# Quarter-array score products, POOL pooling in half pieces and another load order in a fused attention and mixture kernel

## The chip, the cores and the metric

The kernel runs on one core of one Trainium2 chip. The metric is the device time of one execution in microseconds; lower is better. TensorE is called PE here, VectorE DVE, ScalarE ACT, GpSimd POOL; SP is the engine that only issues DMAs.

## What is computed

Three stages follow one another. The sizes are B = 8, H = 8, S = 576 queries and keys, head size 64, keys and values averaged over groups of 8 (72 pooled keys), N = B*S = 4608 tokens of width 512.

```python
k_p, v_p = k.reshape(B,H,72,8,64).mean(3), v.reshape(B,H,72,8,64).mean(3)
attn = softmax((q @ k_p.T) / 8)                      # 1e-9 added to each sum
x = (attn @ v_p)                                     # tokens x 512
logits = x @ phi                                     # 32 slots
d, c = softmax(logits, 0), softmax(logits, 1)        # 1e-9 added to each sum
slot_out = per expert: relu((d.T @ x) @ w1) @ w2     # 8 experts, 4 slots each
x = c @ slot_out
out = (s * relu(x @ w_in)**2 + b) @ w_out            # width 512 -> 2048 -> 512
```

## The kernel before, in words

The program is written by hand, one instruction stream per engine, with semaphores between them. The first part (attention, logits, and the sums over tokens that softmax over tokens needs) runs over 36 **units** of 128 queries by 4 heads (every ninth step holds a **mixed** unit, 64 queries of each of two batches by 8 heads), nine units for each of four **pairs** of batches. It is a pipeline in numbered **steps** `n`; each engine walks the same steps in its own program order. In step n PE does, in this order: the fold of the logits of unit n-5 (L1209), the scores of unit n-1 (L1231, or L1225 if the unit is mixed), the transposes of the queries of unit n (L1264), the logits of unit n-4 (L1292, L1287), the transposes of the weights of unit n-3 (L1305), then what belongs to a pair: turns of pooled keys and values (L1147), the product of the values with phi (L1170, `values_phi`), values back to natural order (L1179), and the sums over tokens (L1334 to L1342, L1352, L1361, L1366), once in two halves for each of 8 batches. L1193 are products whose results nobody reads; they stand only in the last steps.

DVE takes the row maximum of the scores in PSUM (L944, `mx`), sums the exponentials of the unit before (L980, `den`), subtracts the maximum into SBUF (L987, `ex`), takes reciprocals (L991), and pools keys (L897, with a second copy of the result by L901). The scores of the next unit wait for that subtraction (`sx_ready`), as they use the same two PSUM banks. ACT exponentiates and copies PSUM to SBUF: queries (L702), keys (L709), values (L718), weights (L725), transposed attention weights (L799). All turns and the queries share PSUM bank 0, so the queries of a step wait until ACT has kept what was turned in the step before.

POOL normalises a unit (L678, `normalise`; step n takes unit n-2, PE transposes that unit in step n+1) and pools key and value pieces: a first addition halves a piece of 8 rows to 4 (L664, 128x768), a second to 2 (L664, 128x384), and two more write the result twice (L671). `pool_pieces(n)` says which whole pieces POOL takes behind the normalisation of step n; `dve_keys(n)` says which thirds of a key piece DVE takes. A pair has three key and three value pieces of 768 KB; the buffer `kvbuf` holds three of the pieces at a time (RING), in the order of `KV_ORDER`. Per later pair DVE pools two key pieces and POOL one key and three value pieces.

SP issues every DMA in program order (L559 to L600), and a wait before one holds all that follow: a `kvbuf` load waits until the piece three places earlier in `KV_ORDER` is pooled, a load of queries until the transposes have read the buffer. The 2 MB expert matrices stand between them.

Behind the 36 units come the expert products (L1389, L1410), and from about 260 us to the end the last two products (L1439, L1455 to L1457), which the change doesn't touch.

The arrays are named in the order of the streams below. A score product of an ordinary unit and one of the mixed unit read in the code:

```python
last = pe.matmul(bank[S_B[j]][:, KEYS * a:KEYS * (a + 1)], qT[rows, a, :], k_sb[...], ...)        # L1231, rows = 64 of 128
last = pe.matmul(bank[S_B[h % 2]][toks, KEYS * (h // 2):...], qT[rows, h // 2, toks], k_sb[...], ...)  # L1225, toks = 64 of 128
```

## Time and profile before

| | us |
|---|---|
| median of 3 runs (lowest, highest) | 707.23 (701.81, 719.14) |
| the profiled execution | 703.28 |
| its span | 701.4 |
| busy: PE, its weight loads, DVE, ACT, POOL | 667.3, 526.2, 384.2, 326.7, 103.4 |
| mean granted clock of PE, of full speed | 0.976 |

A row of a timeline or of a chain of waits begins with its start and its length in us; then come engine, line, operation, what is written and read (partitions x elements), and how many instructions it merges; in brackets the idle time before it and what ended it. PE shows two records for most products in fp32 and one for a transpose, and the records overlap: the length of a row runs on past the start of the next, so a PE piece is taken from start to start. A table of stretches has the stretch, its length, the busy time of PE, weight loads, DVE, ACT and POOL with their instructions, the granted PE clock (1.00 is 2.4 GHz, 0.50 is 1.2 GHz), the DMA share and GB/s. In the page's slices a digit is tenths busy of one fortieth of the span, 17.5 us.

### The profile page before, as it was taken

What the parts mean: (1) busy time and instruction counts of PE and PEld (TensorE: products, weight loads), DVE (VectorE), ACT (ScalarE), POOL (GpSimd) and SP (SyncE); (2) the same over time, 40 slices, a digit from 0 to 9 for tenths busy, and PEclk for the clock granted to TensorE, in tenths of its full rate; (3) what the DMA queues carried; (4) which work ended last, traced back from release to release, by engine and by line L of the source; (5) the groups of instructions that cost most, each with busy time, mean ns of one, the idle gap of its engine ahead of it and who ended that gap; (6) DMA issues with size and microseconds to landing.
All of it is one profiled execution on the core that took longest, in us unless ns stands there. A gap on an engine that the chain in (4) does not pass through costs nothing.

```text
span 701.4 us, 12092 instructions
## 1 busy us (share of the span) xinstructions
PE 667.3 (95%) x4618; PEld 526.2 (75%) x4618; DVE 384.2 (55%) x631; ACT 326.7 (47%) x607; POOL 103.4 (15%) x106
## 2 busy tenths in 40 slices
PE   6759999999998889999999999999999999999996
PEld 6647788787774335888888888888888888888885
DVE  6437777756534566665445454454554544544542
ACT  1436767776631226554444444444444444444442
POOL 2556565662211000000000000000000000000000
PEclk9778999999999999999999999999999999999999
DMA  9948878555257991001001010010010000100101
GB/s 334 325 124 302 315 268 300 183 158 209 90 215 279 427 428 78 0 1 60 1 10 52 1 40 20 0 60 0 0 60 0 30 30 0 61 0 1 61 0 60
DMA packets 25228, 80.37 MB, mean 115 GB/s; under 512 B 6496, under 2 KB 14688, under 8 KB 22368
## 3 DMA queue, kind: packets, MB, share of 16 engines
q1 hardware_dynamic: 25184, 79.76, 30.8%
q8 instruction: 30, 0.49, 0.3%
q14 instruction: 14, 0.11, 0.0%
HBM read 70.32 MB, written 9.44 MB: 114 GB/s over the span
## 4 chain that ended last, share of the span: by engine, by line
PE 88%; POOL 3%; DVE 3%; DMA 2%; ACT 1%; issue 1%; ACTq 0%; SPq 0%; DVEq 0%; POOLq 0%
PE bank L1455 19%; PE bank L1457 19%; PE bank L1456 19%; PE bank L1305 5%; PE bank L1439 5%; PE bank L1231 4%; PE bank L1264 2%; PE bank L1292 2%; POOL kvbuf L664 2%; PE bank L1389 2%; DMA kvbuf<-in_v_dram 2%; PE bank L1410 2%; PE bank L1334 1%; PE bank L1209 1%; PE bank L1352 1%
## 5 line engine op out<-in xcount | busy, mean ns | idle before, releaser
L1455 PE MATMUL bank<-w_hi,r_hi 128*128 128x512 f32 x576 | 224.2, 389 | 1.4 <-DVE r_lo L1093 1.4
L1457 PE MATMUL bank<-w_hi,r_lo 128*128 128x512 f32 x576 | 224.1, 389 | 0.0
L1456 PE MATMUL bank<-w_lo,r_hi 128*128 128x512 f32 x576 | 224.1, 389 | 0.0
L1087 DVE SCALAR_TENSOR_TENSOR win_sb<-win_sb,sb_col 128x512 f32<-128x512 f32 x144 | 108.5, 753 | 196.8 <-ACT win_sb L840 196.8
L840 ACT ACTIVATE win_sb<-bank 128x512 f32<-128x512 f32 x144 | 86.1, 598 | 217.8 <-PE bank L1439 217.8
L1455 PEld LDWEIGHTS bank<-w_hi,r_hi 128*128 128x128 f32 x576 | 108.1, 188 | 24.4 <-DVE r_lo L1093 2.0
L1457 PEld LDWEIGHTS bank<-w_hi,r_lo 128*128 128x128 f32 x576 | 108.1, 188 | 22.5
L1456 PEld LDWEIGHTS bank<-w_lo,r_hi 128*128 128x128 f32 x576 | 108.1, 188 | 22.4
L1093 DVE SCALAR_TENSOR_TENSOR r_lo<-win_sb,sb_col,r_hi 128x512 fp32r<-128x512 f32 x144 | 107.7, 748 | 1.5 <-ACT r_hi L849 1.5
L849 ACT ACTIVATE r_hi<-win_sb,sb_col 128x512 fp32r<-128x512 f32 x144 | 103.2, 717 | 1.6 <-PE bank L1457 1.6
L1439 PE MATMUL bank<-cT,g_st 128*128 (+1 forms) x144 | 56.4, 393 | 0.0
L799 ACT ACTIVATE aT<-bank 72x512 f32<-72x512 f32 x72 | 39.1, 588 | 29.5 <-PE bank L1305 29.4
L678 POOL TENSOR_TENSOR ex<-ex,den 128x576 f32<-128x576 f32 x36 | 41.3, 1149 | 70.8 <-DVE den L991 70.8
L1305 PE MATMUL bank<-ident,ex 128*72 128x128 f32 x288 | 40.8, 287 | 8.9 <-POOL ex L678 8.9
L1305 PEld LDWEIGHTS bank<-ident,ex 128*72 128x72 f32 x288 | 30.7, 120 | 22.3 <-issue 11.5
L664 POOL TENSOR_TENSOR kvbuf<-kvbuf 128x768 f32<-128x768 f32 (+1 forms) x30 | 42.2, 1406 | 24.2 <-DMA kvbuf<-in_v_dram 17.6
L944 DVE TENSOR_REDUCE mx<-bank 128x8 f32<-128x576 f32 x36 | 27.2, 757 | 30.5 <-PE bank L1231 29.5
L1231 PE MATMUL bank<-k_sb,qT 64*128 64x72 f32 x512 | 37.4, 288 | 0.1
L702 ACT ACTIVATE qT<-bank 128x512 f32<-128x512 f32 x36 | 21.5, 597 | 34.2 <-PE bank L1264 34.0
L1231 PEld LDWEIGHTS bank<-k_sb,qT 64*128 64x128 f32 x512 | 32.7, 196 | 2.4 <-issue 1.0
L1439 PEld LDWEIGHTS bank<-cT,g_st 128*128 128x128 f32 x144 | 26.9, 188 | 6.6 <-DVE g_st L1073 0.8
L897 DVE TENSOR_REDUCE kp<-kvbuf 128x64 f32<-128x512 f32 x24 | 24.2, 1024 | 7.9 <-DMA kvbuf<-in_k_dram 7.9
(137 smaller groups left out, 577.4 us busy)
## 6 DMA issues: line engine op xcount, KB each, us to landing
early_third<-in_moe_w_dram SPq DMA_DIRECT2D x6, 2048.0 KB, 13.4
kvbuf<-in_k_dram SPq DMA_DIRECT2D x12, 768.0 KB, 6.0
kvbuf<-in_v_dram SPq DMA_DIRECT2D x12, 768.0 KB, 5.2
out_dram<-win_sb SPq DMA_DIRECT2D x36, 256.0 KB, 2.3
qbuf<-in_q_dram SPq DMA_DIRECT2D x8, 1024.0 KB, 8.6
early<-in_moe_w_dram SPq DMA_DIRECT2D x4, 2048.0 KB, 10.2
late<-in_moe_w_dram SPq DMA_DIRECT2D x4, 2048.0 KB, 17.4
win_sb<-in_moe_w_in_dram SPq DMA_DIRECT2D x4, 1024.0 KB, 4.8
```

The source lines that it names most:

```text
L664: pool.tensor_tensor(buf[:, :, 0:width], buf[:, :, 0:width], buf[:, :, width:2 * width], ALU.add).then_inc(pool_step, 1)
L678: pool.tensor_tensor(e, e, r, ALU.mult).then_inc(a_ready, 1)
L840: act.activation(r_sb[:, n % 2, :], bank[4 + n % 2][:, :], ACT.Relu).then_inc(r_ready, 1)
L849: act.activation(r2_hi[:, n % 2, :], g_sb[:, n % 2, :], ACT.Identity, bias=sb_col[:, 1:2]).then_inc(hi_ready, 1)
L1087: dve.scalar_tensor_tensor(out=g_sb[:, n % 2, :], in0=r_sb[:, n % 2, :], scalar=sb_col[:, 0:1], in1=r_sb[:, n % 2, :], op0=ALU.mult, op1=A ...
L1093: dve.scalar_tensor_tensor(out=r2_lo[:, n % 2, :], in0=g_sb[:, n % 2, :], scalar=sb_col[:, 1:2], in1=r2_hi[:, n % 2, :].bitcast(F32), op0= ...
L1231: last = pe.matmul(bank[S_B[j]][:, KEYS * a:KEYS * (a + 1)], qT[rows, a, :], k_sb[i % 2][rows, H * bb + HB * unit_half(U) + a, :], start=T ...
L1305: last = pe.transpose(bank[A_B[g]][0:KEYS, P * a:P * (a + 1)], ex[:, U % EXR, HB * g + a, 0:KEYS], ident[:, :])
L1439: pe.matmul(bank[4 + f % 2][:, :], g_st[:, P * f:P * (f + 1)], cT[:, bass.ds(c * CH, CH)], start=True, stop=True).then_inc(h_ready, 1)
L1455: pe.matmul(acc, r2_hi[:, f % 2, toks], w_hi[:, f, :], start=(f == 0), stop=False)
L1456: pe.matmul(acc, r2_hi[:, f % 2, toks], w_lo[:, f, :], start=False, stop=False)
L1457: last = pe.matmul(acc, r2_lo[:, f % 2, toks], w_hi[:, f, :], start=False, stop=(f == F2C - 1))
```

## The change

- **Scores**: each score product of an ordinary unit is split into two with 64 query columns each, so that four products at 64 rows by 64 columns stand in a row, as in the mixed unit.
- **Small products**: the fold of the logits (L1209) and the turn of the token sums (L1352) are split by output partitions too (64 and 64; 64 and 8). The broadcast of the running maximum (L1246) takes all 128 rows instead of 32.
- **Denominator**: the two products with a column of ones (L1340, L1342) go. The matrix of token sums takes the 73rd column of `ex`, which holds 1e-9, with it, and the later step divides by 1e-9.
- **POOL**: a piece is pooled in two parts (`halve`, and `pool_rest` with the other three additions), which stand in different steps, and POOL takes two of the three key pieces of a later pair; DVE pools one.
- **Loads**: `KV_ORDER` is keys then values for every pair; the value pieces of pair 1 are issued ahead of the first matrix.
- **Start**: the last value piece of pair 0 is turned one step later, and its product with phi too, through another PSUM bank.
- **DVE**: two copies from SBUF to SBUF (L901, L1010) are written as reductions over one element.

```diff
         def weights_step(i):
-            return TPP * i + 2 if i else 3
+            return TPP * i + 2 if i else 4
...
-                steps = (2, 3, 4, 5, 6, 6) if i == 1 else tuple(TPP * i - 9 + x for x in (0, 1, 2, 4, 5, 6))
-                at += [(i, 2 * (x // GP), x % GP) for x in range(2 * GP) if steps[x] == n]
+                steps = (3, 4, 4) if i == 1 else tuple(TPP * i - 10 + g for g in range(GP))
+                at += [(i, 0, g) for g in range(GP) if steps[g] == n]
...
-                steps = (3, 5, 6, 8) if i == 1 else tuple(TPP * i - 7 + 2 * x for x in range(4))
-                at += [(i, *((1, 0), (0, 1), (1, 1), (1, 2))[x]) for x in range(4) if steps[x] == n]
+                steps = (3, 4, 4, 5, 5, 6, 6, 7, 7, 8) if i == 1 else tuple(TPP * i - 10 + x for x in range(10))
+                pieces = ((0, 1), (0, 2), (1, 0), (1, 1), (1, 2))
+                at += [(pieces[x // 2][0], i, pieces[x // 2][1], x % 2) for x in range(10) if steps[x] == n]
...
+            for u in range(PIECES):
+                load_kv(1, 1, u)
             load_matrix(0)
-            load_kv(1, 1, 0)
             load_q(1, 0)
             load_q(1, 2)
...
-                dve.tensor_copy(pm[:, 1:, :], pm[:, 0:1, :].to_broadcast([P, QUADS, SLOTS])).then_inc(pm_ready, 1)
+                dve.reduce_max(pm[:, 1:, :], pm[:, 0:1, :].to_broadcast([P, QUADS, SLOTS]).unsqueeze(3), AX.X).then_inc(pm_ready, 1)
...
-                        last = pe.matmul(bank[MISC][:, SLOTS * j:SLOTS * (j + 1)], l4[:, l4_cols(U)][:, P * j:P * (j + 1)], fold[:, 0, :],
-                                         start=True, stop=True)
+                        for half, toks in parts():
+                            first = P * j + HALF * half
+                            last = pe.matmul(bank[MISC][toks, SLOTS * j:SLOTS * (j + 1)], l4[:, l4_cols(U)][:, first:first + HALF],
+                                             fold[:, 0, :], start=True, stop=True)
...
-                                last = pe.matmul(bank[S_B[j]][:, KEYS * a:KEYS * (a + 1)], qT[rows, a, :],
-                                                 k_sb[i % 2][rows, H * bb + HB * unit_half(U) + a, :], start=True, stop=True)
+                                for _, toks in parts():
+                                    last = pe.matmul(bank[S_B[j]][toks, KEYS * a:KEYS * (a + 1)], qT[rows, a, toks],
+                                                     k_sb[i % 2][rows, H * bb + HB * unit_half(U) + a, :], start=True, stop=True)
...
-                    if half == 0:
-                        pe.matmul(found[:, DEN:DEN + 1], dl[:, g % 2, 0:QT, :].rearrange("p j s -> p (j s)"), ones[:, :],
-                                  start=False, stop=True, skip_group_check=True)
-                        last = pe.matmul(found[0:QUAD, DEN:DEN + 1], dl[:, g % 2, QT, :], ones[:, :],
...
-                        last = pe.matmul(bank[B_B][0:KEYS, SLOTS * h:SLOTS * (h + 1)], b_sb[:, h // HB, KEYS * x:KEYS * (x + 1)], fold[:, 0, :],
-                                         start=True, stop=True)
+                        for keys in (slice(0, HALF), slice(HALF, KEYS)):
+                            last = pe.matmul(bank[B_B][keys, SLOTS * h:SLOTS * (h + 1)],
+                                             b_sb[:, h // HB, LANES * x + keys.start:LANES * x + keys.stop], fold[:, 0, :],
```

**POOL, its first normalisations.** In the rows below `ex<-ex,den` is the normalisation of a unit and the others are additions of one piece (`kp` a key piece, `vp` a value piece). Before, a whole value piece stands behind the second normalisation:

```order
L678 TENSOR_TENSOR ex<-ex,den 128x8x72 x2
L664 TENSOR_TENSOR kvbuf<-kvbuf 128x3x256
L664 TENSOR_TENSOR kvbuf<-kvbuf 128x3x128
L671 TENSOR_TENSOR vp<-kvbuf 128x3x64 x2
L678 TENSOR_TENSOR ex<-ex,den 128x8x72 x2
```

Now the first addition of a key piece stands there, and from then on two parts of different pieces between two normalisations:

```order
L677 TENSOR_TENSOR ex<-ex,den 128x8x72 x2
L657 TENSOR_TENSOR kvbuf<-kvbuf 128x3x256
L677 TENSOR_TENSOR ex<-ex,den 128x8x72
L664 TENSOR_TENSOR kvbuf<-kvbuf 128x3x128
L670 TENSOR_TENSOR kp<-kvbuf 128x3x64 x2
L657 TENSOR_TENSOR kvbuf<-kvbuf 128x3x256
L677 TENSOR_TENSOR ex<-ex,den 128x8x72
```

The value piece of pair 1 moved behind both key pieces and two more normalisations.

**PE, steps 3 and 4.** `kp` and `vp` are turned pieces, `k_sb,qT` scores, `qbuf` queries, `ident,ex` transposed weights, `phi_bd,vT` the product with phi, `aT,vphi` logits. Before:

```order
L1147 MATMUL bank<-ident,vp 128x128 x6
L1231 MATMUL bank_2<-k_sb,qT 128x72 x8
L1264 MATMUL bank<-ident,qbuf 128x128 x4
L1305 MATMUL bank<-ident,ex 72x128 x8
L1170 MATMUL bank<-phi_bd,vT 72x64 x8
L1231 MATMUL bank_2<-k_sb,qT 128x72 x8
```

Now:

```order
L1146 MATMUL bank<-ident,vp 128x128 x3
L1235 MATMUL bank_2<-k_sb,qT 64x72 x16
L1268 MATMUL bank<-ident,qbuf 128x128 x4
L1311 MATMUL bank<-ident,ex 72x128 x8
L1146 MATMUL bank<-ident,vp 128x128 x3
L1235 MATMUL bank_2<-k_sb,qT 64x72 x16
L1268 MATMUL bank<-ident,qbuf 128x128 x4
L1169 MATMUL bank<-phi_bd,vT 72x64 x8
L1298 MATMUL bank<-aT,vphi 32x256 x4
```

A score group is 16 products instead of 8; one turn of values and the product with phi moved down, the latter to just ahead of the first logits.

**SP, behind the key pieces of pair 1.** `early` is an expert matrix. Before:

```order
L537 DMA kvbuf<-in_k_dram 128x1536 x3
L557 DMA early<-in_moe_w_dram 128x4096
L537 DMA kvbuf<-in_v_dram 128x1536
L546 DMA qbuf<-in_q_dram 128x8x256
```

Now:

```order
L540 DMA kvbuf<-in_k_dram 128x1536 x3
L540 DMA kvbuf<-in_v_dram 128x1536 x3
L560 DMA early<-in_moe_w_dram 128x4096
L549 DMA qbuf<-in_q_dram 128x8x256
```

The matrix and the next queries moved behind all three value pieces.

## Rows read from the trace of the kernel before

**Rows 1.** The page: span, and the granted clock in 40 slices.

```profile
span 701.4 us, 12092 instructions
...
PEclk9778999999999999999999999999999999999999
```

**Rows 2.** Busy time by stretch: steps 11 to 36, and one pair of batches.

```profile
72.41:190.04 117.63, 117.22 (x1582) 93.69 (x1581) 79.77 (x166) 82.18 (x178) 59.97 (x58) 1.00 0.61 217
82.38:125.13 42.75, 42.58 (x571) 34.25 (x571) 31.23 (x63) 29.94 (x66) 25.58 (x26) 1.00 0.76 267
```

**Rows 3.** The chain of waits, 36 to 49 us.

```profile
36.67 0.93 DVE kp L897
...
37.94 4.49 DMA kvbuf<-in_v_dram
...
42.51 1.80 POOL kvbuf L664
...
44.38 1.00 POOL kvbuf L664
...
45.45 1.13 POOL vp L671 x2
46.59 1.11 POOL ex L678
```

**Rows 4.** Timeline of POOL, 42 us.

```profile
42.51 2.87 POOL L664 TENSOR_TENSOR kvbuf<-kvbuf 128x768 f32<-128x768 f32 x2 [9.73 <-DMA kvbuf<-in_v_dram]
```

**Rows 5.** Timeline of PE: steps 2, 5 and 11.

```profile
26.42 0.90 PE L1147 MATMUL bank<-ident,vp 128*128 128x128 f32 x3 [3.03 <-POOL vp L671]
...
47.75 1.92 PE L1305 MATMUL bank<-ident,ex 128*72 128x128 f32 x8 [8.55 <-POOL ex L678]
...
74.94 1.07 PE L1305 MATMUL bank<-ident,ex 128*72 128x128 f32 x8
```

**Rows 6.** Busy time and clock by stretch, 28 to 60 us.

```profile
28.00:30.00 2.00, 2.00 (x16) 1.87 (x15) 0.65 (x1) 0.71 (x2) 0.00 (x0) 0.50 0.98 313
...
44.00:48.00 4.00, 0.25 (x2) 0.23 (x3) 0.00 (x0) 0.00 (x0) 3.84 (x6) 0.50 0.57 117
...
58.00:60.00 2.00, 2.00 (x22) 1.42 (x21) 1.84 (x3) 1.37 (x4) 1.92 (x2) 1.00 0.74 187
```

**Rows 7.** Timeline of DVE, step 5.

```profile
38.18 0.76 DVE L944 TENSOR_REDUCE mx<-bank 128x8 f32<-128x576 f32 x1 [0.26 <-PE bank L1225]
...
40.18 0.19 DVE L991 RECIPROCAL den<-den 128x8 f32<-128x8 f32 x1
```

**Rows 8.** The page, DMA issues: queries; KB each, us to landing.

```profile
qbuf<-in_q_dram SPq DMA_DIRECT2D x8, 1024.0 KB, 8.6
```

**Rows 9.** Timeline of PE, steps 12 to 16.

```profile
81.12 0.31 PE L1337 MATMUL bank<-ex,dl 128*32 128x72 f32 x8
81.36 0.38 PE L1340 MATMUL bank<-ones,dl 128*128 128x1 f32 x2
...
81.82 0.63 PE L1209 MATMUL bank<-fold,l 128*128 128x32 f32 x4
82.38 1.11 PE L1231 MATMUL bank<-k_sb,qT 64*128 64x72 f32 x16
83.43 0.66 PE L1264 MATMUL bank<-ident,qbuf 128*128 128x128 f32 x4
...
86.77 0.73 PE L1225 MATMUL bank<-k_sb,qT 64*64 64x72 f32 x32
87.43 0.33 PE L1240 MATMUL bank<-ident,pm 128*128 128x128 f32 x1
...
89.92 1.17 PE L1352 MATMUL bank<-fold,b_sb 128*72 128x32 f32 x16
...
97.09 0.63 PE L1264 MATMUL bank<-ident,qbuf 128*128 128x128 f32 x4 [0.17 <-ACT k_sb L709]
```

**Rows 10.** One line of DVE: the copy of the maxima.

```profile
L1010 DVE COPY pm<-pm x8: 226/700/990, 68.3 to 206.9; 128x128 f32<-128x128 f32 x8
```

More of the change, by code:

```diff
@@ L398, in value_bank @@
         def value_bank(i, u):
-            return bank[Q_B if i or u < 2 else B_B]
+            return bank[Q_B]
         def natural_bank(i, half):
@@ L406, in first_query_bank @@
             keys = [(i, u) for i in range(1, PAIRS) for u in range(PIECES) if key_step(i, u) == n]
-            values = [(i, u) for i in range(PAIRS) for u in range(PIECES) if value_step(i, u) == n and (i or u < 2)]
-            weights = [i for i in range(PAIRS) if weights_step(i) == n]
+            values = [(i, u) for i in range(PAIRS) for u in range(PIECES) if value_step(i, u) == n]
+            weights = [i for i in range(1, PAIRS) if weights_step(i) == n]
             naturals = [(i, h) for i in range(PAIRS) for h in range(2) if natural_step(i, h) == n and (i or h == 0)]
@@ L654, in _, with halve, pool_rest @@
                                pattern=[[-1, P]], channel_multiplier=1).then_inc(consts, 1)
-            pool.memset(ones[:, :], 1.0).then_inc(consts, 1)
             pool.memset(phi_bd[:, :, :], 0.0).then_inc(phi_zero, 1)
-            def pool_piece(which, i, u, piece):
+            PARTS = [(which, 0, u, part) for which, u in ((0, 1), (1, 1), (1, 2)) for part in range(2)]
+            PARTS += [part for n in range(STEPS) for part in pool_parts(n)]
+            def halve(which, i, u):
                 slot, loads = kv_piece(which, i, u)
+                buf = kvbuf[:, slot]
                 pool.wait_ge(kv_in[slot], 16 * loads)
+                pool.tensor_tensor(buf[:, :, 0:ROW // 2], buf[:, :, 0:ROW // 2], buf[:, :, ROW // 2:ROW], ALU.add).then_inc(pool_step, 1)
+            def pool_rest(which, i, u):
+                slot, loads = kv_piece(which, i, u)
                 buf = kvbuf[:, slot]
-                for n, width in enumerate((ROW // 2, ROW // 4)):
-                    pool.tensor_tensor(buf[:, :, 0:width], buf[:, :, 0:width], buf[:, :, width:2 * width],
-                                       ALU.add).then_inc(pool_step, 1)
-                    pool.wait_ge(pool_step, 2 * piece + n + 1)
+                pool.wait_ge(pool_step, PARTS.index((which, i, u, 0)) + 1)
+                pool.tensor_tensor(buf[:, :, 0:ROW // 4], buf[:, :, 0:ROW // 4], buf[:, :, ROW // 4:ROW // 2], ALU.add).then_inc(pool_step, 1)
+                pool.wait_ge(pool_step, PARTS.index((which, i, u, 1)) + 1)
                 if i:
@@ L678, in normalise @@
                 pool.tensor_tensor(e, e, r, ALU.mult).then_inc(a_ready, 1)
-            POOLED = [piece for n in range(STEPS) for piece in pool_pieces(n)]
-            pool_piece(0, 0, 1, 0)
-            pool_piece(1, 0, 1, 1)
-            pool_piece(1, 0, 2, 2)
+            for which, u in ((0, 1), (1, 1), (1, 2)):
+                halve(which, 0, u)
+                pool_rest(which, 0, u)
             for n in range(STEPS):
@@ L686, in _ @@
                     normalise(n - 2)
-                for i, which, u in pool_pieces(n):
-                    pool_piece(which, i, u, 3 + POOLED.index((i, which, u)))
+                for which, i, u, part in pool_parts(n):
+                    (halve, pool_rest)[part](which, i, u)
             pool.wait_ge(b_ready, 2 * B)
@@ L1314, in _ @@
                 for i in range(PAIRS):
-                    if n == weights_step(i):
+                    if i and n == weights_step(i):
                         values_phi(i, n)
```

104 lines of the change are left out of this document (50 added, 54 removed).

## The prediction

> **What bounds the kernel now.** I read the page first: a span of 701.4 us, with PE at its full clock except near the start, where the digits fall to 7 and 8 [rows 1]. The part from about 260 us on is not touched. So the question is the first 218 us, and I cut them by stretches. From 72.41 to 190.04 us (steps 11 to 36) PE is busy for 117.22 of 117.63 us at clock 1.00, and in one pair of batches, nine steps, for 42.58 of 42.75 us; DVE has 31.23 us there, ACT 29.94, POOL 25.58 [rows 2]. That stretch is bound by PE: what PE no longer does there is gained, until another engine's round trip takes over.
>
> The beginning is different. The chain of waits shows a DVE reduction of keys at 36.67 us, then a value piece's DMA of 4.49 us, three kinds of POOL additions, and only then, at 46.59, the normalisation that PE needs [rows 3]. POOL had stood idle for 9.73 us for that value piece [rows 4], with the normalisation queued behind it, and PE lost 8.55 us to it [rows 5]. PE also pays afterwards: the clock is 0.50 at 44 to 48 us and 1.00 again at 58 to 60 [rows 6]. A wait of 3.03 us at step 2 [rows 5] is followed in the same way by 0.50 at 28 to 30 us [rows 6].
>
> **Part A, the start (to the transposes of unit 8 in step 11).** The profile of a changed start must be worked out anew along its slowest engine, which I take to be POOL. Up to the scores of unit 4 I give nothing: turning the last value piece one step later takes the wait of 3.03 us out of step 2, but the normalisation of unit 0 still stands behind all three first pieces on POOL, so about 3 us of PE idle and the half clock come back in step 3; and the phi product, now just ahead of the logits that need it, adds one round trip over ACT. So DVE's maximum for unit 4 stays at 38.18 us and its reciprocal ends at 40.18 + 0.19 = 40.4 [rows 7]. From there POOL has no reason to pause: keys 1 and 2 of the pair are loaded by then, and the first value piece, issued when DVE has pooled its keys at about 38, needs 4.49 us to land [rows 3], while POOL reaches it only at 43.7. From the chain a first halving takes 44.38 - 42.51 = 1.87 us, the rest of a piece 46.59 - 44.38 = 2.21, a normalisation 1.11 [rows 3]. Between 40.4 and the release of unit 8 stand six normalisations (3 to 8), the rests of five pieces and the halvings of four: 6 x 1.11 + 5 x 2.21 + 4 x 1.87 = 25.2 us, so unit 8 is released at 65.6 and its transposes start at about 65.7, against 74.94 [rows 5]. Part A gives **9.2 us**. POOL's own work grew here (a key piece of 1.87 + 2.21 = 4.1 us more); the gain is that the DMA wait is gone. Late next is POOL itself.
>
> Bounds of part A. Above: the whole PE wait, 8.55 us, and half of the roughly 10 us at half clock (44 to 56 us), 5 us, and five score groups of 0.39, as derived below: 15.5. Below: the queries of pair 1 are now behind the first matrix and all three value pieces. Value piece 3 waits for key piece 3 to be pooled (40.4 + 1.11 + 2.21 = 43.7), then 0.8 + 2.1 + 1.0 MB follow; at the 313 GB/s of one row [rows 6] that is 12.5 us, and 8.6 us is the median for such a load [rows 8], so they land between 52 and 56. PE wants them at about 54: the normalisation of unit 5 ends at 40.4 + 3 x 1.11 + 2 x 2.21 + 2 x 1.87 = 51.9, and its transposes, a turn and the next scores lie between. The key piece behind them holds DVE for some us too, under POOL's chain. If both break through that cover and the clock falls again, some 5 us go: lower bound 4.
>
> **Part B, steps 12 to 36.** A score group of an ordinary unit takes 83.43 - 82.38 = 1.05 us, the mixed unit's, with the same number of output values and four quarter arrays, 87.43 - 86.77 = 0.66 [rows 9]. The new groups have that form, row halves and column halves in the same order. 22 of the 25 groups here are ordinary: 22 x 0.39 = 8.6 us. Against it: where keys were turned a step earlier, the queries already wait 0.17 us for ACT's copy of them [rows 9], so shorter scores only lengthen that wait. I take that once for each of two pairs, 0.8, and as much again for the other copies that ACT makes out of bank 0: 7.0 us remain. DVE is no hindrance: from its maximum to the end of the subtraction 40.18 - 38.18 = 2.0 us pass [rows 7], while PE has over 3 us of other work in a step of 42.75 / 9 = 4.75 us [rows 2]. POOL would have 9 x 1.11 + 5 x 4.08 = 30.4 us per pair where PE keeps over 38; cover enough.
>
> The products with ones go: 81.82 - 81.36 = 0.46 us for each batch [rows 9], six here: 2.8 us. The column that replaces them lies in products that run anyway. The logits' fold takes 82.38 - 81.82 = 0.56 us [rows 9], 11 double and 3 single ones here, 12.5 in all; the turn of the token sums takes 1.17 at most [rows 9] and, without the overlap of its last record, 1.0, six of them. No row shows these two in their new form. At best they shorten like the scores (by 0.37 of their length): 2.6 and 2.2 us. At worst each of the doubled records takes as long as a present one, which doubles both: a loss of 7 and 6. The nearest row is the column-split group of L1337, 8 records of 72 columns in 81.36 - 81.12 = 0.24 us, 30 ns each [rows 9], against 65 ns for each of the 16 records of an ordinary score group with the same 72 columns; so neighbours in other columns do overlap, and I take a third of the best: 0.9 and 0.7. Part B: 7.0 + 2.8 + 0.9 + 0.7 = **11.4 us**, bounds 5 and 16.
>
> The Trainium skill ("TensorE: Matmul & The Clock Gate", Part 3, The mechanism) says that weight loads overlap running matmuls only where their row groups differ. The two small products keep all 128 rows and split columns only; by that rule nothing is gained on them, and by its reading at its harshest the doubled records are paid in full. The 30 ns of the row above speak against the harsh reading.
>
> **Part C, the last steps and the start's small change.** Two more batches without the ones products: 0.9 us. The copy of the maxima takes 226 to 990 ns [rows 10]; its long cases lie beside POOL additions, and in the last steps PE waits for it. As a reduction I take the short value always and 0.5 us off the path. The remaining folds and turns give 0.4. Part C: **1.8 us**, bounds 0.5 and 3.
>
> The Trainium skill ("SBUF — State Buffer", on the port that DVE and GpSimd share) says the same of the copy: a copy can take the shared port pair and block against GpSimd, a reduction on this chip never does. By it the 0.5 us is safe; without it the copy would have stayed between the two values of the row.
>
> Behind the last steps the expert products wait for matrices whose loads are started by PE's own progress, so the gain passes through. Sum: 9.2 + 11.4 + 1.8 = 22.4; the span becomes 679.0. The profiled execution took 703.28, 1.9 more than its span, so 680.9, rounded to **681 us**. That is 3.2% below its own execution and 3.7% below the median of 707.23; the runs shown reach from 701.81 to 719.14.
>
> **Rivals.**
> 1. *The start gives little.* PE waits for POOL in short pieces all the way and runs them at half clock, or queries land late. For it: every PE wait of 3 us so far was followed by 0.50. Against: the new waits are about 1 us each. Part A falls to 4: 686 us.
> 2. *Another round trip takes the steady steps.* ACT's copies out of bank 0, or DVE, hold every step, or the quarter products with the same keys twice are no faster than halves. For it: the 0.17 us. Against: 1.1 us of other PE work stand in most such places. The 7.0 us go: 688 us.
> 3. *The column-split small products are paid by the record.* 7 + 6 lost instead of 1.6 gained in part B, and 3.5 in part C (two folds and two turns doubled, 3.1, instead of the 0.4): 681 + 18 = 699 us, no difference.
> 4. *POOL is starved again, once per pair.* Three places of the piece buffer and one issue queue: if a load lands a step (4.75 us) later than POOL's program wants it, the normalisation behind it is held as at 42.51. A wait like that cost 8.55 us and about 5 of half clock; in each of pairs 1 to 3 that is 3 x 13.5 = 41 us: 681 + 41 = 722 us, slower. It decides where the wait costs over 22.4 / 3 = 7.5 us per pair. For it: the second key piece of pair 2 can be issued only when a value piece is pooled, one step ahead of its own halving. Against: in pairs 2 and 3 almost all other pieces have two steps, 9 us, for a landing of 4.49.
>
> **How the numbers follow.** Chances: forecast 0.62, rival 1 0.14, rival 2 0.14, rival 3 0.06, rival 4 0.04. The measurement can tell about 2% from no change, so the border is 693 us. The forecast and rivals 1 and 2 lie below it, save a small part at their upper ends; faster 0.86, within 2% 0.10, slower 0.04. The range takes in rivals 1 and 2 with some room, and below the better half of the bounds of A and B: 670 to 693.
>
> **What would show it.** POOL: no wait for a value piece's DMA above 1 us before 60 us, and the transposes of unit 8 at 64 to 68 us. Scores: 0.66 us from start to start in every group. One pair of batches: 42.75 - 4 = 38.5 to 39 us, PE still full, with waits of queries for ACT up to 0.6 us once or twice per pair. Folds below 0.56 and turns of token sums below 1.0 us; above those, rival 3. Copies of the maxima as reductions near 0.25 us. I would be wrong in part A if PE's clock stayed at 0.50 past 45 us or a queries' wait of more than 2 us stood at step 9, and in part B if the pair took more than 41 us.

## The result: no faster, and where the 30 us went

The changed kernel takes 710.79 us (median of 14 runs, 706.79 to 715.48); the kernel before took 702.92 on the same chip (14 runs, 699.43 to 719.14). The ratio of the two is 1.012, with a 95% interval of 1.009 to 1.014: slower, by less than the 2% that stood as the border. Three of the 14 executions of the kernel before (714 to 719 us) are slow ones, at a lower clock, such as any kernel shows now and then; the ratios here and below leave them out. The forecast was 681, range 670 to 693. The profiled execution of the changed kernel is its slowest, 715.48 us with a span of 713.7, so the two traces lie 12.3 us apart where the medians lie 7.9 apart; the stretches below carry that excess.

I cut both traces, and the forecast, at the same four places. Starts in us, from the timelines of PE; the third column is the forecast's own arithmetic (74.94 - 9.2, then the stretches of before less 11.4 and 1.8).

| | before | after | forecast |
|---|---|---|---|
| transposes of unit 8 (step 11) | 74.94 | 70.40 | 65.7 |
| scores of step 36 | 190.04 | 193.53 | 169.4 |
| first expert product | 218.26 | 229.72 | 195.8 |
| end of the span | 701.4 | 713.7 | 679.0 |

So the start gained 4.5 us instead of 9.2, the steady steps lost 8.0 instead of gaining 11.4, the last steps lost 8.0 instead of gaining 1.8, and the rest is longer by 0.8 (483.98 us instead of 483.14). The page of the changed kernel shows the new trouble in one line; it answers to [rows 1], and a digit is one fortieth of 713.7 us:

```profile
span 713.7 us, 13446 instructions
...
PEclk9896999999795999999999999999999999999999
```

In the kernel before the clock had been full from the fifth slice on. Now there is a 6 in the fourth, a 7 at 178 to 196 us and a 5 at 214 to 232, and the windows below find more. They answer to [rows 2, 6] and have the same columns (the clock is the third number from the end):

```profile
44.00:48.00 4.00, 2.59 (x80) 1.98 (x78) 2.42 (x5) 2.64 (x6) 4.00 (x5) 1.00 0.99 419
...
60.00:68.00 8.00, 6.14 (x60) 4.35 (x62) 6.99 (x15) 3.51 (x8) 7.21 (x7) 0.50 0.94 360
70.40:193.53 123.13, 119.64 (x1998) 88.93 (x1994) 67.91 (x151) 80.66 (x174) 61.26 (x60) 0.93 0.56 195
95.00:105.00 10.00, 10.00 (x182) 7.17 (x185) 4.03 (x8) 7.11 (x15) 5.03 (x5) 0.83 0.27 82
175.00:185.00 10.00, 10.00 (x134) 7.60 (x137) 3.00 (x7) 3.71 (x10) 2.04 (x2) 0.63 0.25 104
193.53:229.72 36.19, 34.99 (x381) 25.69 (x377) 9.81 (x30) 9.56 (x24) 5.52 (x5) 0.80 0.47 175
```

At 44 to 48 us, where the kernel before waited at clock 0.50, PE now works at 1.00: the wait for the value piece is gone. But 60 to 68 us is at 0.50, and the stretch from step 11 to 36, which had 1.00 throughout, has a mean of 0.93. PE is listed as busy for the whole of 175 to 185 us while it runs at a mean of 0.63. A busy PE is not a quick PE.

The instruction that costs the most is found by walking PE's timeline from start to start, as in [rows 9]:

```profile
103.42 0.31 PE L1212 MATMUL bank<-fold,l 128*64 128x32 f32 x4
103.66 0.73 PE L1235 MATMUL bank<-k_sb,qT 64*64 64x72 f32 x32
104.32 0.66 PE L1268 MATMUL bank<-ident,qbuf 128*128 128x128 f32 x4
...
106.81 3.17 PE L1357 MATMUL bank<-fold,b_sb 128*64 128x32 f32 x32
109.90 0.29 PE L1235 MATMUL bank<-k_sb,qT 64*64 64x72 f32 x4
```

Scores take 104.32 - 103.66 = 0.66 us, as forecast. The turn of the token sums takes 109.90 - 106.81 = **3.09 us** (3.10 in others) where it took 1.0 to 1.1 before; its 32 records come every 97 ns, against 69 ns for each of the 16 before. (Its row names only the first of its two shapes.) There are eight such turns: five in the steady stretch, three in the last steps. The forms of line L1357, and who waits for it:

```profile
L1357 PE MATMUL bank<-fold,b_sb x256: 193/222/317, 84.2 to 225.2; 128*64 128x32 f32 x64, 128*8 128x32 f32 x64
...
  ACT bT L766: 22.2, 8
```

The last of the eight even runs at half clock and takes 225.37 - 220.89 = 4.5 us.

The other small products did well: the fold of the logits takes 0.35 us for a double one (99.51 - 99.16, below) instead of 0.56, and the half-sums that had carried the products with ones take 0.75 instead of 1.21:

```profile
97.81 1.20 PE L1340 MATMUL bank<-ex,dl 128*32 128x292 f32 x8
98.79 0.44 PE L1345 MATMUL bank<-ex,dl 128*32 128x73 f32 x8
99.16 0.42 PE L1212 MATMUL bank<-fold,l 128*64 128x32 f32 x8
99.51 0.73 PE L1235 MATMUL bank<-k_sb,qT 64*64 64x72 f32 x32
...
102.67 0.70 PE L1340 MATMUL bank<-ex,dl 128*32 128x292 f32 x8
103.18 0.31 PE L1345 MATMUL bank<-ex,dl 128*32 128x73 f32 x8
103.42 0.31 PE L1212 MATMUL bank<-fold,l 128*64 128x32 f32 x4
```

(0.75 is 103.42 - 102.67; the group at 97.81 falls partly into a half-clock stretch.)

At the start, POOL's wait of 9.73 us [rows 4] and PE's of 8.55 [rows 5] are gone, and others stand in their place. From the timelines of PE, DVE and POOL, 55 to 62 us:

```profile
55.25 1.11 PE L1268 MATMUL bank<-ident,qbuf 128*128 128x128 f32 x4 [4.89 <-DMA qbuf<-in_q_dram]
...
61.86 1.24 PE L1235 MATMUL bank<-k_sb,qT 64*64 64x72 f32 x32 [1.99 <-DVE ex L986]
```

```profile
58.59 1.03 DVE L896 TENSOR_REDUCE kp<-kvbuf 128x64 f32<-128x512 f32 x1 [10.83 <-DMA kvbuf<-in_k_dram]
```

```profile
60.50 1.81 POOL L657 TENSOR_TENSOR kvbuf<-kvbuf 128x768 f32<-128x768 f32 x1 [5.29 <-DMA kvbuf<-in_k_dram]
```

Three engines wait for a transfer at once: PE for the queries of step 9, DVE and POOL for the first key piece of pair 2. DVE's wait is not idle time that costs nothing: the subtraction of step 9's scores is queued behind that reduction, and the 1.99 us of PE is for it. All three transfers stand behind the first 2 MB matrix on the one issue queue.

### The profile page after: what moved, and what is told of

It is laid out like the page before. It is cut to its first block, busy times and chain, and to the rows that moved or that the text cites. A ratio compares the mean times of both kernels' runs of the same rounds, so it can differ in the third digit from the quotient of the medians.

```text
span 713.7 us, 13446 instructions
## 1 busy us (share of the span) xinstructions
PE 679.6 (95%) x5298; PEld 523.6 (73%) x5298; DVE 372.0 (52%) x619; ACT 326.9 (46%) x607; POOL 114.7 (16%) x117
## 4 chain that ended last, share of the span: by engine, by line
PE 84%; DMA 7%; DVE 3%; POOL 2%; issue 2%; ACT 1%; ACTq 0%; DVEq 0%; POOLq 0%
PE bank L1461 18%; PE bank L1462 18%; PE bank L1463 18%; PE bank L1445 4%; PE bank L1311 4%; DMA late<-in_moe_w_dram 4%; PE bank L1357 4%; PE bank L1298 2%; PE bank L1235 2%; PE bank L1268 2%; DMA kvbuf<-in_k_dram 2%; PE bank L1395 2%; PE bank L1340 2%; PE bank L1194 1%; POOL kvbuf L657 1%
## 5 line engine op out<-in xcount | busy, mean ns | idle before, releaser
L1311 PE MATMUL bank<-ident,ex 128*72 128x128 f32 x288 | 43.1, 299 | 2.2 <-POOL ex L677 2.2
L1268 PE MATMUL bank<-ident,qbuf 128*128 128x128 f32 x144 | 26.1, 310 | 11.8 <-DMA qbuf<-in_q_dram 8.0
L657 POOL TENSOR_TENSOR kvbuf<-kvbuf 128x768 f32<-128x768 f32 x18 | 32.6, 1811 | 15.7 <-DMA kvbuf<-in_k_dram 10.6
L1235 PE MATMUL bank<-k_sb,qT 64*64 64x72 f32 x1024 | 25.8, 242 | 3.2 <-DVE ex L986 3.0
L1268 PEld LDWEIGHTS bank<-ident,qbuf 128*128 128x128 f32 x144 | 18.2, 160 | 14.3 <-DMA qbuf<-in_q_dram 8.4
```

Source lines behind the costliest of these rows:

```text
L1235: last = pe.matmul(bank[S_B[j]][toks, KEYS * a:KEYS * (a + 1)], qT[rows, a, toks], k_sb[i % 2][rows, H * bb + HB * unit_half(U) + a, :], s ...
L1268: last = pe.transpose(bank[Q_B][:, P * a:P * (a + 1)], src, ident[:, :])
L1311: last = pe.transpose(bank[A_B[g]][0:KEYS, P * a:P * (a + 1)], ex[:, U % EXR, HB * g + a, 0:KEYS], ident[:, :])
```

## The experiments

Twelve kernels, in four groups of runs: 1 to 4, 5 to 8, 9 to 11, and 12. Each ratio is to the kernel before in the same group (medians of 701.0, 703.1, 702.5 and 702.9 us). As these medians differ by 2 us, kernels of two groups are compared more safely by their ratios. Two theories stood at first: the split turn costs the time, by itself and by the clock behind it; or the start does, since its waits leave half clock behind them. Behind each stands what was expected of it, as it was written before the run.

**1. a_turn_whole: the turn of the token sums as one product again, all else as changed**

```diff
-                        for keys in (slice(0, HALF), slice(HALF, KEYS)):
+                        for keys in (slice(0, KEYS),):
```

> The changed kernel, but the turn of the token sums is one product of 72 output rows again (with the new column stride). Theory 1, the split turn costs 2.1 us for each of eight batches (3.10 against 1.01 us from start to start), and the low clocks that follow it cost more: the turn takes 1.0 us, eight turns give back 17 us, the stretches at 0.50 behind turns go too, 2 to 6 us; run 688 to 692 us where the changed kernel is at 710.8. Rival, the turn only fills time in which PE would wait for something else (POOL, ACT) anyway: under 8 us come back, run above 703.

684.86 us (683.85 to 686.33), ratio 0.978 (0.974 to 0.982). One line of the code is worth 25.9 us between the medians, 24 by the ratios (1.012 - 0.978 of 702.9). Timeline of PE and windows (steps 11 to 36; the last steps):

```profile
99.82 1.17 PE L1357 MATMUL bank<-fold,b_sb 128*72 128x32 f32 x16
100.92 0.73 PE L1235 MATMUL bank<-k_sb,qT 64*64 64x72 f32 x32
```

```profile
67.55:172.38 104.83, 101.92 (x1918) 78.67 (x1914) 67.95 (x151) 80.37 (x174) 61.44 (x60) 1.00 0.66 234
...
172.38:198.27 25.89, 23.44 (x333) 18.25 (x329) 9.80 (x30) 9.59 (x24) 5.53 (x5) 0.99 0.62 229
```

The steady stretch falls from 123.13 to 104.83 us and its clock rises from 0.93 to 1.00; the last steps fall from 36.19 to 25.89, the clock from 0.80 to 0.99. The five turns of the steady stretch, 2.0 us each, are 10.0 of its 18.3; PE's waits for "issue" (below) fall from 2.3 to 0.9, 1.4 more; the other 7 are left for the stretches at half clock, which are gone with the split turn though no other instruction differs. The clock column allows at most (1 - 0.93) x 123.13 = 8.6 us for them. The low clock went with the turn.

**2 and 3. a_turn_grouped and a_turn_32: the same split in another order, and in pieces of 32, 32 and 8 rows**

```diff
-                    for h in range(H):
-                        x = h % HB
-                        for keys in (slice(0, HALF), slice(HALF, KEYS)):
+                    for keys in (slice(0, HALF), slice(HALF, KEYS)):
+                        for h in range(H):
+                            x = h % HB
```

> The changed kernel, the same 16 split products of the turn, but first all eight with 64 output rows, then all eight with 8. Theory 1a, what costs is the change between a 64-column and an 8-column piece at each product (97 ns per record): with one change left the turn takes 0.5 to 0.9 us and the run is at 687 to 692. Rival 1b, each doubled record that fills all 128 rows costs by itself, because its weight load cannot run under a product in the same rows: the turn stays at 3.1 us, the run at 711. Rival 1c, the 8-column pieces are slow in themselves: about half of the loss stays, turn 1.8 to 2.4 us, run 698 to 704.

688.15 us (687.59 to 689.84), ratio 0.982 (0.979 to 0.985).

```diff
-                        for keys in (slice(0, HALF), slice(HALF, KEYS)):
+                        for keys in (slice(0, QUAD), slice(QUAD, HALF), slice(HALF, KEYS)):
```

> The changed kernel, the turn in three parts of 32, 32 and 8 output rows, alternating as before, 48 records. Theory 1a, the cost lies in the change of piece size between 64-column and 32-column tiles, and 8 columns count as a 32-column tile: no change is left, the turn takes 0.7 to 1.3 us, run 688 to 693. Rival 1b (records cost by themselves, 97 ns): 48 x 97 = 4.7 us, run 724. Rival 1c (8 columns slow in themselves): turn 2 us or more.

685.86 us (684.65 to 686.96), ratio 0.978 (0.975 to 0.982). PE's timelines, of the grouped kernel first:

```profile
102.07 1.68 PE L1357 MATMUL bank<-fold,b_sb 128*64 128x32 f32 x32
103.68 0.73 PE L1235 MATMUL bank<-k_sb,qT 64*64 64x72 f32 x32
```

```profile
100.70 0.70 PE L1357 MATMUL bank<-fold,b_sb 128*32 128x32 f32 x48
101.33 0.73 PE L1235 MATMUL bank<-k_sb,qT 64*64 64x72 f32 x32
```

The same 32 records take 3.10 us when pieces of 64 and 8 columns alternate and 1.61 us when all of one width come first; in 32, 32 and 8, as many as 48 records take 0.63 us, 13 ns each. So neither the number of records nor the split as such is dear: the alternation of 64 with 8 is. The grouped order saves 1.49 us and has one change of width where the other has fifteen, so a change costs about 1.49 / 14 = 0.11 us. That is an estimate, which takes it that the records cost the same otherwise. The grouped turn itself took longer than the 0.5 to 0.9 us expected of it, 50 ns a record, and that no run explains. The pieces of 32, 32 and 8 alternate too and pay nothing of the kind; the reading that fits all three is that 8 and 32 columns use the array in the same division and 64 and 8 do not. It is argued from these three orders; no run tries other pairs of widths.

The Trainium skill ("TensorEngine Tiling (Array Packing)", Tiling Modes, Key Properties) says that a change of tiling mode, not of the tile within one, drains the engine; the three orders agree with it, and add the price. Another sentence of it ("TensorE: Matmul & The Clock Gate", Part 3, The mechanism), that a weight load overlaps running products only where its row groups differ, does not agree: 13 ns per record was measured among products that all use the same 128 rows, and the weight loads of kernel 3's turns are 85 to 113 ns long each, so in a turn of 0.63 us they must overlap.

**4. a_queries_first: the queries of pair 1 ahead of the first matrix, the split turn kept**

```diff
-            load_matrix(0)
             load_q(1, 0)
             load_q(1, 2)
+            load_matrix(0)
```

> The changed kernel with the queries of pair 1 issued ahead of the first expert matrix instead of behind it; the split turn stays. Theory 2, the matrix of 2 MB held up the queries (PE idle 4.89 us at 50 us) and, less, the first key piece of pair 2 (DVE idle 10.83 us): the wait for queries goes, that for the key piece stays in part since the matrix is still ahead of it; 2 to 5 us come back, run 706 to 709. Rival, DMA bandwidth is the limit whatever the order: queries wait less, the key piece waits as long or longer, under 1 us comes back.

708.77 us (702.53 to 711.18), ratio 1.010 (1.004 to 1.017): within the 706 to 709 expected, but it can't be told from 710.79. PE's wait for the queries of step 9 is gone, and its wait for DVE grew to take its place:

```profile
61.80 1.24 PE L1235 MATMUL bank<-k_sb,qT 64*64 64x72 f32 x32 [6.04 <-DVE ex L986]
```

DVE still waits 9.5 us for its key piece of pair 2. Unit 8's transposes start at 70.03, against 70.40. Of two transfers that are late together, moving one gives nothing that these runs can measure.

**5. b_turn_split: the kernel before, with only the turn of the token sums split**

```diff
-                        last = pe.matmul(bank[B_B][0:KEYS, ...], b_sb[:, h // HB, KEYS * x:KEYS * (x + 1)], fold[:, 0, :],
-                                         start=True, stop=True)
+                        for keys in (slice(0, HALF), slice(HALF, KEYS)):
+                            last = pe.matmul(bank[B_B][keys, ...], b_sb[:, h // HB, KEYS * x + keys.start:KEYS * x + keys.stop], fold[:, 0, :],
+                                             start=True, stop=True)
```

> The kernel before with one thing of the change: the turn of the token sums split into 64 and 8 output rows, alternating. Theory 1, the alternation costs by itself, whatever else is changed: the turn goes from 1.0 to 3.1 us, eight of them are 17 us, and low clocks behind it add 2 to 8: 720 to 726 us where the kernel before is at 701 to 703. Rival, it costs only beside the new scores (whose pieces are 64 by 64): turn 1.0 to 1.5 us, under 705.

735.31 us (731.46 to 742.43), ratio 1.048 (1.039 to 1.058): some 30 us (28.3 between the two profiled spans), more than the 19 to 25 expected. The turn is the same as in the changed kernel, and so is what follows:

```profile
109.43 3.17 PE L1353 MATMUL bank<-fold,b_sb 128*64 128x32 f32 x32
112.53 1.12 PE L1231 MATMUL bank<-k_sb,qT 64*128 64x72 f32 x16
```

```profile
60.00:190.00 130.00, 129.61 (x1520) 100.29 (x1519) 78.38 (x163) 79.88 (x170) 62.63 (x60) 0.91 0.60 207
```

Eight turns at 2.0 us are 16; a clock of 0.91 where it was 1.00 carries the rest, (1 - 0.91) x 130 = 11.7 us. PE has hardly a wait there that could be blamed: 0.9 us in all between 60 and 225 us. The clock is 0.74 at 89.4 to 96 us, 0.58 at 138 to 146, 0.54 at 162 to 176 and 0.69 at 190 to 201, each directly behind a split turn; behind the turn that ends at 112.53 it is 1.00. Taken from the changed kernel the split gives about 25 back, added to the one before it costs about 30: one cause, seen from both sides.

**6. b_scores: the kernel before, with only the quarter scores**

```diff
-                                last = pe.matmul(bank[S_B[j]][:, KEYS * a:KEYS * (a + 1)], qT[rows, a, :],
-                                                 k_sb[i % 2][rows, H * bb + HB * unit_half(U) + a, :], start=True, stop=True)
+                                for _, toks in parts():
+                                    last = pe.matmul(bank[S_B[j]][toks, KEYS * a:KEYS * (a + 1)], qT[rows, a, toks],
+                                                     k_sb[i % 2][rows, H * bb + HB * unit_half(U) + a, :], start=True, stop=True)
```

> The kernel before with the quarter-array scores alone. Theory, the scores are worth 0.39 us in each of 32 ordinary groups, less where ACT or POOL ends the step: 7.0 of 8.6 us in steps 12 to 36 and up to 1.5 at the start: 692 to 695 us. Rival, another engine's round trip takes the place of the shorter scores: above 698.

694.74 us (694.52 to 696.08), ratio 0.988 (0.983 to 0.993): 8.4 us from the scores alone. In the steady stretch, 71.47 to 182.46 us, it is 115.1 - 111.0 = 4.1; PE's own busy time there fell by 7.3, and its waits grew from 0.4 us to 3.6; the longest:

```profile
PE bank L1265 <- DMA qbuf<-in_q_dram: 1.8, 1, 1.8
PE bank L1265 <- ACT k_sb L709: 1.1, 2, 0.6
```

The other half of the gain lies in the start, 3.5 us, and the last steps.

**7. c_matrix_later: turn in 32s, queries first, and the first matrix behind the key pieces of pair 2**

```diff
-            load_matrix(0)
             load_q(1, 0)
             load_q(1, 2)
             for i in range(2, PAIRS):
                 for u in range(PIECES):
                     load_kv(0, i, u)
+                if i == 2:
+                    load_matrix(0)
                 load_matrix(2 * i - 3)
```

> The changed kernel with the turn in parts of 32, 32 and 8, and the first expert matrix issued behind the key pieces of pair 2, so behind the queries of pair 1 too. Theory 2, the 2 MB of the matrix make both waits at step 8 and 9 (queries 2.8 to 6.6 us, key piece 10 us, which in its turn holds DVE and so the scores): with the matrix away the piece has only the queries before it, DVE's wait falls below 4 us, PE's below 1.5, and the half clock that follows goes: 5 to 9 us below the 685.9 of the turn in 32s, 677 to 681. Rival, the piece is late because its place in the buffer comes free late (issued at 48 us, wanted at 48): DVE still waits 5 us or more and under 3 us come back.

684.78 us (684.19 to 687.58), ratio 0.974 (0.969 to 0.980). Unit 8's transposes start at 62.45 instead of 68.81 in kernel 3, and yet, where 5 to 9 us were expected, the time differs by only 1.1 us between the medians and 2.7 by the ratios: of the 6.4 us, 3.5 are left at step 36 (173.15 against 176.64) and 2.8 in the span (682.4 against 685.2). DVE's wait for the key piece fell from 10.31 to 4.32 us, short of the theory's 4; and PE now waits 3.65 us for POOL ahead of the transposes at 78.81.

**8. c_whole_pieces: the same, with POOL pooling whole pieces**

```diff
-                steps = (3, 4, 4, 5, 5, 6, 6, 7, 7, 8) if i == 1 else tuple(TPP * i - 10 + x for x in range(10))
+                steps = (3, 3, 4, 4, 5, 5, 6, 6, 7, 7) if i == 1 else tuple(TPP * i - 10 + x // 2 * 2 for x in range(10))
```

> As the run before, but POOL pools each piece whole behind one normalisation (4.1 us in one go, every second step) instead of in two parts. Theory, halves only keep a normalisation from waiting 2 us in places where PE has less than that in hand: in steps of about 4 us one unit in two is late by up to 1 us for 27 steps, 2 to 8 us slower than with the halves. Rival, the order of the loads did all the work and halves are worth nothing: same within 1.5 us.

685.85 us (684.13 to 692.33), ratio 0.978 (0.970 to 0.985): not to be told from kernel 7, where 2 to 8 us more were expected. PE waits 6.0 us for POOL between 40 and 75 us instead of 2.9, and unit 8 is later by 0.9. The two parts of a piece give nothing that can be measured.

**9. d_whole_later: kernel 7 with the turn whole**

> The changed kernel with the turn of the token sums whole and the first expert matrix behind the key pieces of pair 2. In the changed kernel with the whole turn the transposes of unit 8 start at 67.6 us, with the matrix moved at 62.5. Theory, PE's program has become long enough for its time that it now and then waits for its own instructions (gaps ended by nothing but issue, six in the run with 48 records per turn, one with 16, none before), and these gaps ate the 5 us in the run with the matrix moved: with 16 records per turn there are at most two such gaps and the 5 us stay: 679 to 682 us. Rival, gaps come with the faster start whatever the number of records: four gaps or more, 683 to 686.

683.76 us (681.41 to 686.28), ratio 0.974 (0.968 to 0.980). The edits are that of kernel 1 and the move of the matrix in kernel 7. Unit 8 starts at 61.88, and the scores of step 36 at 174.24: later than in kernel 1, which had started 5.7 us after it. PE waits 3.65 us for POOL at 78.08, with half clock behind it, and has only 0.35 us of "issue". So it is not that the gaps of kernel 7 ate the start's gain; the stall had moved, and kernel 7 has the same one. The 679 to 682 expected did not come, nor did the rival's four gaps.

**10. d_keys_step9: the same, DVE takes its first third of the keys of pair 2 a step later**

```diff
-                steps = (3, 4, 4) if i == 1 else tuple(TPP * i - 10 + g for g in range(GP))
+                steps = (3, 4, 4) if i == 1 else (9, 9, 10) if i == 2 else tuple(TPP * i - 10 + g for g in range(GP))
```

> As the run before, and DVE pools the first third of the first key piece of pair 2 in step 9 instead of step 8. Theory, DVE's wait of 4.3 us for that piece (landing at 52.3 us) is a wait of a program that asks too early; one step later it has landed: DVE's wait under 0.5 us, PE's wait of 0.86 for the scores goes, 0.5 to 2 us faster than the run before. Rival, DVE then has two thirds in step 9 beside the maxima and holds the next scores instead: same or slower.

684.08 us (683.13 to 686.25), ratio 0.976 (0.971 to 0.980). DVE's wait is gone and the time is the same. POOL and PE show why:

```profile
74.70 1.80 POOL L658 TENSOR_TENSOR kvbuf<-kvbuf 128x768 f32<-128x768 f32 x1 [7.34 <-DMA kvbuf<-in_v_dram]
```

```profile
77.66 1.92 PE L1312 MATMUL bank<-ident,ex 128*72 128x128 f32 x8 [3.77 <-POOL ex L678]
```

The piece that POOL waits for is a value piece of pair 2, and it now stands behind two matrices, 4 MB.

**11. d_fold_whole: kernel 9 with the fold of the logits whole again**

```diff
-                        for half, toks in parts():
-                            first = P * j + HALF * half
-                            last = pe.matmul(bank[MISC][toks, SLOTS * j:SLOTS * (j + 1)], l4[:, l4_cols(U)][:, first:first + HALF],
-                                             fold[:, 0, :], start=True, stop=True)
+                        last = pe.matmul(bank[MISC][:, SLOTS * j:SLOTS * (j + 1)], l4[:, l4_cols(U)][:, P * j:P * (j + 1)], fold[:, 0, :],
+                                         start=True, stop=True)
```

> As the first run of this call, with the logits' fold as one product of 128 output rows again instead of 64 and 64. By the traces the split fold takes 0.36 us where the whole one took 0.56 (double ones) and 0.24 against 0.34 (single ones), 16 and 4 of them: 16 x 0.20 + 4 x 0.10 = 3.6 us, less where a step's end is set by ACT: 2 to 3.6 us slower than the first run of this call. Rival, only its records shrink and the steps are set elsewhere: same within 1 us.

683.85 us (682.68 to 689.14), ratio 0.976 (0.969 to 0.983), against 683.76. The split fold is 0.2 us shorter in each step, and the 2 to 3.6 us that this should give are not seen; runs that spread over 6 us would not show one or two.

**12. e_one_matrix: kernel 10 with the matrices issued one at a time**

```diff
-                if i == 2:
-                    load_matrix(0)
-                load_matrix(2 * i - 3)
+                if i > 2:
+                    load_matrix(i - 2)
                 load_q(i - 1, 1)
                 for u in range(PIECES):
                     load_kv(1, i, u)
-                load_matrix(2 * i - 2)
                 load_q(i, 0)
                 load_q(i, 2)
+                load_matrix(0 if i == 2 else 2)
             load_q(PAIRS - 1, 1)
+            load_matrix(3)
+            load_matrix(4)
```

> d_keys_step9 with the expert matrices issued one at a time between the pieces of keys, values and queries of pairs 2 and 3, so that the value piece of pair 2 no longer lies behind two matrices (4 MB). Theory (a matrix ahead of a piece is what the engines wait for at the start): POOL's wait of 7.3 us for the value piece of pair 2 near 75 and TensorE's 3.8 us behind it fall under 2 us, the stretch of half clock behind them goes, and the time is 3 to 6 us below the 684.1 of d_keys_step9: 678 to 681. Rival (the start's transfers only choose which piece is late; the data wanted by then is the same): the wait comes back at a later pair or at the expert products' matrices, and the time is within 2 us of d_keys_step9, 682 to 686.

**679.98 us** (677.53 to 680.83), ratio 0.966 (0.964 to 0.969): the fastest of all, 22.9 us below the kernel before and 30.8 below the changed one. No engine waits for a piece of pair 2 any more; POOL's waits from 60 to 90 us are for DVE's reciprocals, 2.15 us at most. Page and windows (the steady stretch, the last steps):

```profile
span 679.0 us, 13190 instructions
...
PEclk9699999999988999999999999999999999999999
```

```profile
64.25:169.28 105.03, 101.83 (x1918) 78.60 (x1914) 67.96 (x151) 80.29 (x174) 62.71 (x61) 1.00 0.75 274
169.28:195.16 25.88, 23.43 (x332) 18.24 (x328) 9.79 (x30) 9.56 (x24) 5.52 (x5) 0.99 0.63 230
```

Unit 8 starts here at 64.25, later than in kernels 9 and 10 (61.88, 61.03); what counts is that nothing stalls behind it. The matrices were not late at the expert products: PE waits 1.55 us for DVE ahead of the first, as in the kernel before.

## Why the prediction was wrong, step by step

**Part B, the turn of the token sums: the step that failed.** I took this edit at a gain of 0.7 us, a third of the best case, and named as its worst a loss of 6, "each of the doubled records takes as long as a present one". Measured, a doubled record takes 97 ns and not 69, the turn 3.10 us and not 2.2, and eight of them cost 16 us before the clock is counted; with it, about 25 to 30 us (kernels 1 and 5). The bound was not a bound. I had assumed that a record can't get longer when its product gets smaller, and my "nearest row", the products of L1337, all have the same width of 32 columns; a split of 72 rows into 64 and 8 has a change of width in every second product, which no row of the trace had. Rival 3 named the place and had the sign, 0.06 of the chance and a price of 18 us; its mechanism (paid by the record) is not what was measured, as 48 records of width 32 and 8 take 0.63 us.

**The clock as a consequence of a busy PE.** The prediction reckoned with half clock behind waits only. In the changed kernel 150 to 160 and 175 to 185 us show 0.83 and 0.63 with PE busy throughout, both directly behind a split turn, and the kernel with the turn whole shows 1.00 in these steps. (Not every turn has it behind it: the clock is 1.00 in the 7 us and more behind those that end at 87.30, 109.90 and 133.72.) (The 0.83 of 95 to 105 us stands behind the 2.11 us gap told of below.) No term and no rival held this; together with that gap's share it is some 7 of the 18.3 us in the steady stretch.

**Part B, the rest.** Scores at 0.66 us everywhere: right. Their 7.0 us in the steady stretch were 4.1 alone (kernel 6); 1.8 of the difference was a transfer of queries that the shorter steps no longer hid, which the new order of loads takes away. The fold fell to 0.35 us, better than forecast, the products with ones went for 1.21 - 0.75 = 0.46 each, as read from before. With the turn whole, the steady stretch takes 104.8 us where 115.1 - 11.4 = 103.7 was forecast: the sum without that one term stood, by 1.1 us. The fold's share of it is not seen in the time (kernel 11).

**Part A, the start.** The forecast was 9.2 us, the gain 4.5, close to the lower bound of 4 and by the mechanism named there: queries and a key piece behind the first matrix, "if both break through that cover and the clock falls again". They did, 4.89 and 10.83 us, and 55 to 68 us ran at 0.50. I had put the landing of the queries at 52 to 56 and PE's wish for them at about 54; steps 3 to 8 went quicker than that (PE asked at 50.4), so the cover was thinner. It was rival 1, with the POOL chain right: it does run in normalisations, rests and halvings of about 5.1 us a step once the data is there (kernel 12: 45.35, 50.41, 55.46, 60.53). With the loads in order unit 8 starts at 64.25, 10.7 us earlier than before. The start moves by 2.8 us between kernels that are equal up to there (67.55 in kernel 1, 70.31 in kernel 2, 70.40 after), so 4.5 has that uncertainty.

**Part C.** The forecast was 26.4 us for the last steps; with the turn whole they take 25.9. Three of the eight turns lie here; I had counted six in part B where there are five. The copy of the maxima as a reduction takes 285 to 290 ns in all eight cases, where the copy took 226 to 990 [rows 10]: even, as forecast, and 0.04 longer.

**Rivals 2 and 4** did not come: ACT holds the queries 0.56 us at most (twice in kernel 6, once in the changed one), and POOL is not starved once per pair. But one wait of rival 4's kind, for one value piece of pair 2, came up as soon as the start was mended (kernels 9 and 10) and took back about 4 us.

**The forecast as a whole.** For the kernel that the change meant to be, 681 us was near: 684.9 with one line put back. That 680.0 came with the loads mended as well is in part luck, since that order of loads was not in the forecast and the terms differ from it (scores 4.1 alone and not 7.0, no gain seen from the fold, 10.7 instead of 9.2 at the start). The measured 1.2% slower lies in the band within 2%, which I gave 0.10 (rival 3 had 0.06); that was far too little, since rival 3 had no price for a form that no row showed. The new start was never run without the other changes, so its share is read from traces alone.

## What to carry to other kernels

When a product on TensorE is split by output columns, split it so that neighbours use the array in the same division (32, 32 and 8, or 64 and 64); pieces of 64 and 8 in turn cost about 0.1 us at each change here, and the clock behind them. A nearest row gives a bound only if it has the form of what the change makes, neighbours included; "no worse than now per record" is a guess until a row shows it. On one issue queue, a large transfer ahead of small ones is late for whoever comes next: here moving one piece moved the stall and spreading the large ones removed it, and a start quicker by 6 us gave 1 to 3 us until the next stall was gone.

## What was not expected of the hardware

- **The price of a change of width**: 97 ns per record alternating 64 and 8 columns, 50 ns grouped, 13 ns in 32, 32 and 8, 69 ns whole (72 columns).
- **Half clock behind a busy PE.** From 177.42 us in the changed kernel the records show half speed (scores 1.24 us instead of 0.73) directly behind a split turn. The clock is 1.00 from 165 to 177 us, PE busy for 12.00 of 12.00, the turn among it:

```profile
165.00:177.00 12.00, 12.00 (x189) 8.72 (x187) 6.37 (x16) 8.12 (x16) 3.45 (x3) 1.00 0.46 166
```

```profile
174.33 3.17 PE L1357 MATMUL bank<-fold,b_sb 128*64 128x32 f32 x32
177.42 0.55 PE L1212 MATMUL bank<-fold,l 128*64 128x32 f32 x8
177.90 1.24 PE L1235 MATMUL bank<-k_sb,qT 64*64 64x72 f32 x32
```

In kernel 9 the same speed stands behind a wait, as [rows 5, 6] had it. What of the split turn brings it on no run tells apart.

- **Gaps with no releaser.** The changed kernels have gaps on PE that end in "issue", of which the kernel before has none; in the changed kernel one of 2.11 us, in kernel 3, which with kernels 7 and 8 has the most PE instructions, six of together 5.6 us:

```profile
94.33 0.63 PE L1268 MATMUL bank<-ident,qbuf 128*128 128x128 f32 x4 [2.11 <-issue]
```

```profile
PE bank L1235 <- issue: 2.3, 2, 1.4
PE bank L1367 <- issue: 1.6, 1, 1.6
PE bank L1250 <- issue: 1.1, 1, 1.1
PE bank L1357 <- issue: 0.4, 1, 0.4
PE bank L1212 <- issue: 0.2, 1, 0.2
```

The page's instruction queue grows with them, from 30 packets before to 36 after and 37 in kernel 3. That these gaps are waits for the program itself to be fetched would fit both, but no run here tells it apart; they are not what decides the time, as kernels 7 (3.5 us of them) and 9 (0.35 us) can't be told apart.
